# Unused expert slots spread over the slot sequence, halves of neighbouring slots interleaved

## The reference

```python
x = attention(q, k, v, w_phi)          # linear attention with exp features, 32 heads
h = x @ moe_w_in                       # 512 -> 2048
x = (h * clip(h + 3, 0, 6) / 6) @ moe_w_out
logits = x @ moe2_w_gate               # 8 experts, each token goes to one of them
e = argmax(logits)
out = softmax(logits)[e] * sigmoid(x @ moe2_w_output_gate)[e] * (relu(x @ w1[e]) @ w2[e])
```

## Time and profile before

| | |
|---|---|
| median of 3 runs | 962.37 us (957.13 to 965.53) |
| profiled execution | 964.04 us, span 962.5 us, mean granted clock 0.959 |
| PE busy | 869.5 us (90%), 7480 matmuls |
| DVE, ACT, POOL busy | 580.6, 388.8, 74.9 us |
| L834, w1 of the slots | 125.9 us, x2112 (22 slots of 96) |
| L846, w2 of the slots | 117.5 us, x528 (22 slots of 24) |
| instruction queue q8 | 41 packets, 0.67 MB |

### The profile page before, as it was taken

One profiled execution on the slowest core, in us unless ns is written; L12 is line 12 of the kernel. 1 busy time (PEld: TensorE's weight loads), 2 busy tenths in 40 slices (PEclk: granted clock), 3 DMA queues, 4 the chain that ended last, 5 costly groups with the idle time before them and its releaser, 6 DMA issues.

```text
span 962.5 us, 20311 instructions
## 1 busy us (share of the span) xinstructions
PE 869.5 (90%) x7480; PEld 574.2 (60%) x7481; DVE 580.6 (60%) x1202; ACT 388.8 (40%) x666; POOL 74.9 (8%) x120
## 2 busy tenths in 40 slices
PE   5999999998899999997999999992499999999990
PEld 3777777777455555553555555552377777777770
DVE  3778788875795987985987987545131322222223
ACT  2445456656456565664656665522010100011011
POOL 1000000000000001001001001011011111111111
PEclk9999999999999999998999999995599999999995
DMA  6243344331565366465266452554317342664110
GB/s 191 92 161 113 132 160 161 128 123 36 192 235 202 143 234 223 162 230 216 97 226 224 156 206 121 201 182 150 103 46 299 137 162 98 228 251 176 44 34 13
DMA packets 44062, 151.36 MB, mean 157 GB/s; under 512 B 7710, under 2 KB 12062, under 8 KB 37856
## 3 DMA queue, kind: packets, MB, share of 16 engines
q1 hardware_dynamic: 38320, 134.14, 39.2%
q0 software_dynamic: 5520, 16.31, 4.9%
q10 hardware_dynamic: 160, 0.07, 0.0%
HBM read 104.72 MB, written 47.21 MB: 158 GB/s over the span
## 4 chain that ended last, share of the span: by engine, by line
PE 57%; PEld 14%; DVE 10%; issue 8%; DMA 4%; PEldq 3%; ACT 2%; SPq 1%; DVEq 0%; POOL 0%; POOLq 0%; ACTq 0%
PE ps L743 19%; PE ps L732 17%; PEld ps L834 10%; PE ps L607 4%; PE ps L634 4%; PE ps L673 3%; PEld ps L846 3%; DVE arena L1087 3%; PE ps L834 2%; PE ps L648 2%; DVE arena L1094 2%; PE ps L846 2%; DMA arena<-split 1%; DVE u_mx L1253 1%; PE ps L661 1%
## 5 line engine op out<-in xcount | busy, mean ns | idle before, releaser
L732 PE MATMUL ps<-arena,w_in_sb 128*128 128x384 f16 x1152 | 203.5, 329 | 6.0 <-issue 6.0
L743 PE MATMUL ps<-w_out_sb,arena 128*128 128x512 f16 x576 | 172.3, 381 | 9.1 <-DVE stage L1341 9.1
L732 PEld LDWEIGHTS ps<-arena,w_in_sb 128*128 128x128 f16 x1152 | 111.4, 99 | 81.7 <-issue 9.2
L1067 ACT ACTIVATE w_in_sb<-ps 128x512 f16<-128x512 f32 x50 | 29.5, 597 | 257.0 <-PE ps L834 241.3
L834 PEld LDWEIGHTS ps<-w_in_sb,arena 128*128 128x128 f16 x2112 | 124.0, 100 | 9.8 <-issue 5.0
L834 PE MATMUL ps<-w_in_sb,arena 128*128 128x128 f16 x2112 | 125.9, 223 | 4.3 <-DMA arena<-split 2.4
L846 PE MATMUL ps<-arena,w_in_sb 128*128 128x512 f16 x528 | 117.5, 379 | 0.0
L743 PE MATMUL ps<-w_out_sb,stage 128*128 128x512 f16 x288 | 109.7, 381 | 0.0
L1442 DVE SCALAR_TENSOR_TENSOR w_in_sb<-ps,w_in_sb 128x512 f16<-128x512 f32 x50 | 34.3, 691 | 113.7 <-ACT w_in_sb L1067 113.7
L743 PEld LDWEIGHTS ps<-w_out_sb,arena 128*128 128x128 f16 x576 | 55.9, 98 | 68.9 <-issue 11.7
L1033 ACT ACTIVATE arena<-relu 128x384 f16<-128x384 f32 x96 | 50.2, 523 | 106.6 <-DVE relu L1336 106.6
(11 more groups left out here) (175 smaller groups left out, 927.5 us busy)
## 6 DMA issues: line engine op xcount, KB each, us to landing
arena<-in_moe_w SPq DMA_DIRECT2D x16, 2048.0 KB, 13.1
split<-arena SPq DMA_DIRECT2D x16, 2048.0 KB, 7.4
arena<-split SPq DMA_DIRECT2D x32, 1024.0 KB, 5.8
arena<-in_qkt SPq DMA_DIRECT2D x15, 576.0 KB, 6.2
stage<-in_moe_w_in SPq DMA_DIRECT2D x16, 512.0 KB, 4.3
stage<-in_moe_w_out SPq DMA_DIRECT2D x16, 512.0 KB, 5.4
w_in_sb<-rows POOLq DMA_DIRECT2D x25, 257.0 KB, 3.0
arena<-in_v SPq DMA_DIRECT2D x32, 128.0 KB, 4.5
```

Source lines behind the costliest of these rows:

```text
L732: last = nc.tensor.matmul(ps[:, HB[f % GB], 0:BN], w_in_sb[:, lw, c, f * P:(f + 1) * P], xt[:, a, c, lx, :], start=c == 0 and lw + lx == 0 ...
L743: last = nc.tensor.matmul(ps[:, YB + r, :], g_sb[lg_][:, f % GB, r * P:(r + 1) * P], w_out_sb[:, lw, f, :], start=f == 0 and lg_ + lw == 0 ...
```

## The change

The change concerns the expert stage alone.

- **Order of slots.** With u unused slots, the positions 2, 5, 8, ... (each third one, u of them) are the unused ones. Here that is 2, 5 and 8. The 25 positions then hold the experts 0 0 - 0 1 - 2 2 - 2 2 3 3 3 4 4 5 5 6 6 6 6 6 7 7. DVE makes the tables accordingly.
- **Words.** One word for each slot holds need * 4 + parity * 2 + used; TensorE reads it once in `flags`, and takes it apart with register arithmetic.
- **Order on TensorE.** `step(s)` reads the words of slots s-1 and s, then does w1 of slot s, the transposes of s+1, and w2 of slot s-1. DVE's order and POOL's follow.
- **Weights.** SP loads both halves of w1 of expert e once the last slot of e-2 is through w1 (`free_w1`), then both halves of w2 once it is through w2 (`free_at`).

```diff
@@ sync @@
             for e in range(2, E):
                 free = sp.value_load(free_at[0:1, e:e + 1], min_val=1, max_val=SLOTS + 1)
+                free1 = sp.value_load(free_w1[0:1, e:e + 1], min_val=1, max_val=2 * SLOTS + 1)
+                sp.wait_ge(eh_done, free1)
+                for half in range(2):
+                    load_expert(e, 0, half)
                 sp.wait_ge(eo_done, free)
                 for half in range(2):
-                    for m in range(2):
-                        load_expert(e, m, half)
+                    load_expert(e, 1, half)
@@ gpsimd @@
-            step(nc.gpsimd.iota(iota_s[:], [[1, SLOTS], [0, E]], ...))
+            step(nc.gpsimd.iota(iota_s[:], [[1, SLOTS]], ...))
+            step(nc.gpsimd.iota(third_s[:], [[1, SLOTS // 3 + 2], [0, 3]], ...))
+            step(nc.gpsimd.memset(gap_s[:], float(SLOTS + 1)))
+            step(nc.gpsimd.iota(gap_s[:, 2:SLOTS:3], [[1, SLOTS // 3]], base=1, ...))
...
+            next_load(0, 0)
             with pool.Fori(0, (SLOTS - 3) // 2) as i:
                 for a in range(2):
-                    next_load(i * 2 + a, a)
+                    next_load(i * 2 + (a + 1), 1 - a)
                     store(i * 2 + a, a)
-            next_load(SLOTS - 3, 0)
@@ tensor @@
             ranks(BLOCKS - 1, True)
+            pe.drain().then_inc(eh_done, 1)
...
-            def slot(s, a, turn, more=True):
-                parity = pe.value_load(slot_par[0:1, bass.ds(s, 1)], min_val=0, max_val=1)
-                used = pe.value_load(slot_used[0:1, bass.ds(s, 1)], min_val=0, max_val=1)
-                need = pe.value_load(slot_need[0:1, bass.ds(s, 1)], min_val=32, max_val=32 * E)
+            def flags(s):
+                code = pe.value_load(slot_code[0:1, bass.ds(s, 1)], min_val=4 * 32, max_val=4 * 32 * E + 3)
+                return pe.snap(code // 2 % 2), pe.snap(code % 2), pe.snap(code // 4)
+
+            def first_half(s, a, turn, held, more=True):
+                parity, used, need = held
                 pe.wait_ge(ew1_loaded, need)
                 pe.wait_ge(xgt_ready, s + 1)
                 with pe.If(used):
...
                     pe.drain().then_inc(eh_done, 2)
                 if more:
                     slot_transposes(s + 1, 1 - a, turn + a)
+
+            def second_half(s, a, held):
+                parity, used, need = held
                 pe.wait_ge(ew2_loaded, need)
...
+            def step(s, a, turn, more=True):
+                before, now = flags(s - 1), flags(s)
+                first_half(s, a, turn, now, more)
+                second_half(s - 1, 1 - a, before)
+
             slot_transposes(0, 0, 1)
-            slot(0, 0, 1)
-            slot(1, 1, 1)
+            first_half(0, 0, 1, flags(0))
+            step(1, 1, 1)
             with pe.Fori(0, (SLOTS - 3) // 2) as i:
-                slot(i * 2 + 2, 0, i + 2)
-                slot(i * 2 + 3, 1, i + 2)
-            slot(SLOTS - 1, 0, SLOTS // 2 + 1, False)
+                step(i * 2 + 2, 0, i + 2)
+                step(i * 2 + 3, 1, i + 2)
+            step(SLOTS - 1, 0, SLOTS // 2 + 1, False)
+            second_half(SLOTS - 1, 0, flags(SLOTS - 1))
@@ vector @@
+            link(nc.vector.tensor_scalar(unused[:], cnt[:, src, E - 1:E], -1.0, float(SLOTS), ALU.mult, ALU.add))
+            nc.vector.tensor_scalar(slot_gap[:], gap_s[:], unused[:, 0:1], float(2 * SLOTS), ALU.is_le, ALU.mult)
+            link(nc.vector.scalar_tensor_tensor(out=slot_at[:], in0=third_s[:, 1:SLOTS + 1], scalar=unused[:, 0:1], in1=iota_s[:],
+                                                op0=ALU.min, op1=ALU.subtract))
+            link(nc.vector.tensor_tensor(slot_at[:], slot_gap[:], slot_at[:], ALU.subtract))
...
             with dve.Fori(1, (SLOTS - 3) // 2) as i:
+                slot_lo(i * 2 + 1, 1)
+                slot_in(i * 2 + 2, 0)
+                slot_out(i * 2, 0, i)
+                slot_lo(i * 2 + 2, 0)
+                slot_in(i * 2 + 3, 1)
+                slot_out(i * 2 + 1, 1, i)
```

More of the change, by code:

```diff
@@ L144, in moe_program @@
         slot_scale = table(SLOTS)
-        slot_par, slot_used, slot_need, parity_i, slot_row, slot_token = (table(SLOTS).bitcast(I32) for _ in range(6))
+        parity_i, slot_row, slot_token = (table(SLOTS).bitcast(I32) for _ in range(3))
+        slot_at, slot_gap, slot_count = (table(SLOTS) for _ in range(3))
+        slot_code = table(SLOTS).bitcast(I32)
         og_token = table(2).bitcast(I32)
@@ L175, in moe_program @@
         free_at = sb("free_at", [P, E], I32)
+        free_w1 = sb("free_w1", [P, E], I32)
+        unused = sb("unused", [P, 1])
+        unused_before = sb("unused_before", [P, E])
         expert8 = sb("expert8", [P, E])
@@ L1391, in _ @@
             nc.vector.tensor_copy(padrow[:], base[:, 0, :]).then_inc(pad_ready, 1)
[L1392 to L1393 removed]
+            counts = cnt[:, 3, :]
+            link(nc.vector.tensor_tensor(counts, base[:, 0, :], start8[:], ALU.subtract))
+            link(nc.vector.tensor_scalar(cnti[:], counts, float(P - 1), None, ALU.add))
             link(nc.vector.tensor_scalar(cnti[:], cnti[:], P.bit_length() - 1, None, ALU.logical_shift_right))
@@ L1410, in _ @@
[L1410 to L1415 removed]
+            expert, offset, row = slr[:, 0, :], slr[:, 1, :], slr[:, 2, :]
@@ new lines, in _ @@
+            link(nc.vector.scalar_tensor_tensor(out=row, in0=expert, scalar=float(REGION), in1=offset, op0=ALU.mult, op1=ALU.add))
+            nc.vector.tensor_scalar(slot_row[:], row, float(DUMMY), None, ALU.min)
+            nc.vector.tensor_scalar(slot_gap[:], expert, float(E), None, ALU.is_lt)
+            nc.vector.tensor_copy(parity_i[:], expert)
+            link(nc.vector.tensor_scalar(cnti[:, 2:E], cnt[:, src, 0:E - 2], -1.0, 0.0, ALU.add, ALU.max))
+            link(nc.vector.tensor_scalar(cnti[:, 2:E], cnti[:, 2:E], 1, None, ALU.logical_shift_right))
@@ new lines, in _ @@
+            link(nc.vector.tensor_copy(unused_before[:, 2:E], cnti[:, 2:E]))
+            nc.vector.tensor_tensor(slot_count[:], expert, slot_gap[:], ALU.mult)
+            nc.vector.tensor_scalar(parity_i[:], parity_i[:], 1, None, ALU.bitwise_and)
+            link(nc.vector.scalar_tensor_tensor(out=unused_before[:, 2:E], in0=unused_before[:, 2:E], scalar=unused[:, 0:1],
+                                                in1=cnt[:, src, 0:E - 2], op0=ALU.min, op1=ALU.add))
+            nc.vector.tensor_scalar(slot_count[:], slot_count[:], 128.0, 128.0, ALU.mult, ALU.add)
```

70 lines of the change are left out of this document (36 added, 34 removed).

## The result

The changed kernel takes 966.06 us in the median of 8 runs (965.25 to 969.46); the kernel before, run beside it, takes 962.16 (957.13 to 965.53, 8 runs). The ratio is 1.005, with a 95% interval of 1.003 to 1.007: slower by half a per cent, inside the 1% that the prediction called no change, and 1 us from its 965. By these medians the change costs 3.9 us. The profiled execution took 965.41 us with a span of 963.8, at a mean clock of 0.970 (0.959 before).

The account below looks back on a forecast made before the run. TensorE was taken to bound the expert stage, so only its idle places could win. Savings of 4.0, 14.7 and 0.6 us against added costs summed to +1.8 us: 965 us forecast, range 955 to 973.

Parts of the forecast that it names:

- Weights: At expert 2's first w1: earlier loads remove the 2.36 us stall and 1.64 us of slow clock, -4.0 us.
- End: From the last used w2 to the span's end: 9.9 us instead of 24.6, as a used slot is last, -14.7 us.
- Start: Between slot 0's transposes and its w1: one word read instead of three, w1 at 688.5 instead of 689.12, -0.6 us.
- Filling: Ahead of w1 of slot 1, no longer covered by w2 of slot 0: TensorE idle for 2.1 us.
- (A): An empty slot's w1 is a drain: transposes start cold, branches to the w2 behind are exposed; 0.8 us each, +2.4 us.
- the jump at slot 2: First empty slot in the loop: its branch over w1 jumps over code not yet run, +1.6 us exposed.
- (B): An empty slot's w2 is a drain: the next step's words are read with the queue empty; 2.5 us each, +7.5 us.
- The clock: After the filling and the three (B) gaps the clock falls to 1.2 GHz, 1.64 us each, all four taken, +6.6 us.
- Rival (c): Instruction loading decides: waits for code at slots 2 and 4 and in the last step, 974 to 976 us; chance 0.13.
- Rival (b): The (B) gaps are absent, as words and branches are read ahead of the drain: 950 or 948 us; chance 0.08.
- Rival (a): The clock holds after the gaps and the code is there: 957.6 us, by the median 956; chance 0.24.
- Rival (d): Expert 2's loads are still late, so at most 4 us come back: 968 us; no chance of its own, inside forecast's range.

Follow-up runs that it names:

- e1: The kernel before with only w1 of each expert loaded early, both halves first and freed by w1; 956.82 us, ratio 0.995.
- e11: The changed kernel with 64 unused matmuls ahead of the expert stage, moving its code by 128 instructions, half a packet; 973.80 us in one execution.
- e2: The changed kernel with its empty slots back at the end, positions 22 to 24; order of halves, one word and loads as changed; 963.80 us, ratio 1.003.
- e3: The kernel before with its empty slots at positions 2, 5 and 8; order of halves, words and loads as before; 964.79 us, ratio 1.003.
- e7: The changed kernel with short matmuls in place of the drains, 36 of them in an empty w2; 963.83 us, ratio 1.004.
- e12: The changed kernel with 128 unused matmuls ahead of the expert stage, moving its code by 256 instructions, one packet; 965.46 us in one execution.
- e4: The changed kernel with one or two matmuls of 128 columns in place of each drain, results unused; 963.88 us, ratio 1.003.
- e10: The kernel before with early w1, empty slots at 5, 8 and 11, one word, POOL's new order, matmuls for drains, 36 fillers; 958.39 us, ratio 0.998.
- e6: The changed kernel with its empty slots at positions 5, 8 and 11 in place of 2, 5 and 8; 969.91 us, ratio 1.009.
- e8: The kernel before with early w1 loads and empty slots at positions 5, 8 and 11, three words and drains; 960.41 us, ratio 0.998.

## Why the prediction was right

The total was right, 965 for 966.06, and so was the story: what the empty slots cost in the middle is about what they cost at the end. Its points in turn:

- **Weights, -4.0.** Right in mechanism and size, shown alone by e1.
- **End, -14.7.** Right, -14.6.
- **Start, -0.6.** Wrong: 2.84 for 2.92 us. The word is read by 685.4, but DVE's copy ends at 686.36, 1.81 us behind the start of the transposes, and the first matmul comes 1.03 us after it, where the prediction had 0.6. That w1 of slot 0 ran 1.3 us shorter was not foreseen; it is the clock's, and e11 had 8.13 us there with the same order. It is no property of the change.
- **Filling, +2.1.** Right in place and cause; 2.6 of idle time, in e2 as well, with its slow w1. As at the start, the part behind DVE's copy was too cheap: it ends at 696.34 and w1 starts 1.10 us later.
- **(A), +2.4, and the jump at slot 2, +1.6.** 4.3 for 4.0, but by another branch. The jump over w1 did not wait (0.44 us); the one ahead of w2 took 1.12 us and the rest is the drain. e3, e7 and e11 show at slot 2 the 3.5 us that were read from slot 24, so the row was the right bound; that the place of the code decides whether it is paid is what e11 and e12 suggest.
- **(B), +7.5.** Right in place and cause, 8.9 us between starts, 8.4 of idle time. The prediction had DVE's copy as a second way that would hold w1 for 2.1 us by itself; e4 measured it at 2.2.
- **The clock, +6.6.** The mechanism was right, its size was off by 3.7 us: after gaps of 2.92 and 2.50 us it held, after 2.99 and after the filling's 2.60 it fell. The step that failed is to have taken all four from two rows of 2.1 and 2.36 us. The bounds, 0 and 6.6, did hold it.
- **Three instructions more in the loop, "without a price".** Wrong, and the one item of that list that had a price: 2.05 us over the ordinary slots. What counts is where they stand. The words of the slot before are taken apart and its branches run between w1 and the w2 behind it: in the step of slot 13 the sequencer is through with w1 at 819.17 and with this work at 820.45, 1.28 us where before takes 0.78 (810.49 to 811.27). The matmuls still queued and the transposes cover less than that, and w2 now starts 0.57 us after the transposes began. e2 has the same without an empty slot, and e10 (order of before, one word) has 0.45.
- **The last step, +1.35.** Rival (c) had a wait there, of 3.38 us. It came at 1.38, and at 1.12 at slot 2: small pieces of rival (c) in the forecast's case. Its large waits did not come, and no run shows two of them in the changed order; e11, one execution at 973.8, has one and mostly slow clock.

So two errors nearly cancel, and that is luck: the clock, 3.7 us too dear, against slots, last step, (B) and filling, 5.4 us too cheap; and the first w1's 1.3 us, which the change did not bring, helped the total. Rival (b) is refuted by the gaps. Rival (a) held for two of the three gaps and not for the filling. Rival (d) is refuted by the missing stall at slot 6.

What a drain costs is not cleanly shown: a kernel with matmuls in its place has longer code too, so e4, e7 and e10 change two things at once. What stays open is when a gap of 2.1 to 3.4 us lowers the clock: it did after one of three in the changed kernel, in e4 and in e12, after two of three in e6, and after all three in e3, e8 and e11; ahead of w1 of slot 1 it did after a gap of 2.60 us in the changed kernel and did not after 2.59 us in e12. After the six gaps of 0.77 to 1.70 us in e7 and e10 it never did, but two stops of 1.07 and 0.75 us close together in e2 lowered it. Since a kernel's profile is of one execution, the share for each kernel is not known.

## What to carry over

An empty step in the middle of a pipeline takes away the cover under which the sequencer reads words and branches ahead; price it at those, at the next engine's copy and at the clock before moving it there. With (A), (B) and clock together the three slots cost 5.2, 3.8 and 5.6 us here. Split a change into its parts: here the early loads of w1 and a swapped load and store in POOL's list were worth 0.7% by themselves, and the rest of the change lost them. Where the code has branches, look at their own rows before putting a difference of some 3 us down to anything else: in e7 and e11 a branch of 0.4 us became one of 3.8 and 3.6 us with nothing but the length of the code changed up to it, in one traced execution each.

## What the runs showed of the hardware

**A branch that waits for code has a price of its own.** It was 3.38 us before, and 3.46, 3.42, 3.56, 3.58, 3.75, 3.78 and 3.80 in the experiments, 5.84 once, and 0.7 to 2.8 at other places. That these are waits for code can be read from the start and landing of the instruction queue's packets in the traces: all 18 branches of the stage over 0.7 us, in 13 of the 14 kernels, end 1.35 to 1.50 us after such a packet landed (before: it starts at 948.29, lands at 949.21, and the branch that began at 947.25 ends at 950.63). The stops of 1.07, 1.40 and 1.78 us within the transposes of e2, e4 and e6 end 1.40 to 1.47 us after one. In the eight waits of 3.38 to 3.80 us the packet starts 0.91 to 1.04 us after the branch began; in the eight of 0.71 to 1.48 us it was already on its way. The branches of 0.43 to 0.47 us end 2.0 us or more after the last packet, so they are no such waits. A long wait came with 36 fillers in the loop (e7, e10), and with half a packet of padding, where with a whole packet the waits stayed within 0.4 us of the changed kernel's (e11, e12, one execution each).

**A loop of 1067 instructions, once through, waits no more.** This is the expert loop. In the changed kernel the instruction queue moved packets in two windows of the stage, 685 to 740 and 935 to 960 us; its rows there (packets, MB, share of 16 engines):

```profile
q8 instruction: 8, 0.13, 0.9%
```

```profile
q8 instruction: 2, 0.03, 0.7%
```

Between 740 and 935 us it moved none, so the loop stays in. The Trainium skill ("Runtime: NRT & Kernel Launch", Instruction fetch mechanics) gives two figures for what TensorE holds, 128 KiB in one sentence and two lines of 16 KiB in another. With the page's 256 instructions to 16 KiB the loop is 67 KB, an estimate; the trace agrees with the first figure and not with the second. The dense layer's loop does wait where it goes round: the 4.68 us of the earlier trace rows end 1.37 us after a packet that landed at 449.98.

**Register work between matmuls is hidden only by what is queued ahead of it.** With the queue empty the load of the second word starts 0.75 us after that of the first (rows of L869, 724.38 and 725.13), of which 0.30 us are the load. Under w2 the reading of words is free in both orders. Taking them apart again and branching ahead of w2, with only the rest of w1 and eight transposes queued, cost 0.12 us in each slot.
